# An attention and feed-forward kernel: the high part of two score tiles as two 64-row matmuls, and relu squared in place

## The reference, cut to what matters

```
scores = (1/3136) * z @ z.T            # z: 3136 x 64
attn   = maximum(scores, 0) ** 2
x      = u * (attn @ v)                # v, u: 3136 x 256
h      = maximum(x @ w_in, 0)          # w_in: 256 x 1024
conv   = sum over 3 taps of conv_w[k] * h shifted by k - 1
y      = (h * sigmoid(conv)) @ w_out   # w_out: 1024 x 256
```

## Time and profile before

| what | value |
|---|---|
| median of 2 runs | 1743.33 us (1741.52 to 1745.14) |
| the profiled execution | 1742.73 us |
| its span, first to last instruction | 1740.9 us |
| mean granted TensorE clock | 0.996 |
| matmuls, each with a weight load of its own | 8232 |
| TensorE busy | 1701.0 us |
| DVE, ACT, POOL busy | 1372.0, 1218.1, 196.8 us |

### The profile page before, as it was taken

How to read it: one execution, slowest core, us unless ns; L and a number is a source line. 1 busy time by engine, 2 the same in 40 slices (tenths; PEclk the granted TensorE clock), 3 DMA queues, 4 the chain that set the end, 5 groups by cost and what they waited for, 6 DMA issues and landing times.

```text
span 1740.9 us, 22661 instructions
## 1 busy us (share of the span) xinstructions
PE 1701.0 (98%) x8232; PEld 1548.7 (89%) x8232; DVE 1372.0 (79%) x1826; ACT 1218.1 (70%) x2022; POOL 196.8 (11%) x145
## 2 busy tenths in 40 slices
PE   8899999999999999999999999999999999999996
PEld 7799999988999999998899999999889999999995
DVE  7687778789877878788887788778888777878784
ACT  7667767777776676677777666767776776776664
POOL 7200000024000000003300000000420000000000
PEclk9999999999999999999999999999999999999998
DMA  5100000032000000003200000000310000000000
GB/s 147 53 27 1 27 27 1 27 93 74 1 27 27 1 27 27 27 1 106 62 1 28 27 27 1 27 27 6 112 50 27 1 27 27 1 27 27 22 1 21
DMA packets 28093, 55.34 MB, mean 32 GB/s; under 512 B 2896, under 2 KB 13648, under 8 KB 27984
## 3 DMA queue, kind: packets, MB, share of 16 engines
q1 hardware_dynamic: 27984, 53.90, 10.0%
HBM read 41.04 MB, written 12.85 MB: 31 GB/s over the span
## 4 chain that ended last, share of the span: by engine, by line
PE 88%; DVE 5%; ACT 2%; issue 1%; DMA 0%; POOL 0%; ACTq 0%; DVEq 0%; POOLq 0%
PE ps_h L325 15%; PE ps_av L302 14%; PE ps_av L301 14%; PE ps_av L300 14%; PE ps_y L338 14%; PE ps_s L282 7%; PE ps_s L283 7%; DVE g_sb L583 1%; DVE g_lo L603 1%; DVE attn_lo L544 1%; DVE g_sb L591 1%; PE ps_av L304 1%; PE ps_av L305 1%; ACT attn_hi L410 1%; DMA w_raw<-w_all 0%
## 5 line engine op out<-in xcount | busy, mean ns | idle before, releaser
L556 DVE SCALAR_TENSOR_TENSOR attn<-ps_s,relu_s 128x448 f32<-128x448 f32 x672 | 411.8, 617 | 237.2 <-ACT relu_s L415 236.8
L300 PE MATMUL ps_av<-attn_lo,v_hi 128*128 128x448 f32 x1344 | 494.6, 368 | 10.2 <-DVE attn_lo L544 7.9
L302 PE MATMUL ps_av<-attn_hi,v_lo 128*128 128x448 f32 x1344 | 494.9, 368 | 0.0
L301 PE MATMUL ps_av<-attn_hi,v_hi 128*128 128x448 f32 x1344 | 494.4, 368 | 0.0
L415 ACT ACTIVATE relu_s<-ps_s 128x448 f32<-128x448 f32 x672 | 358.3, 539 | 147.9 <-PE ps_s L283 147.7
L544 DVE TENSOR_TENSOR attn_lo<-attn,attn_hi 128x896 fp32r<-128x896 f32 x336 | 374.7, 1115 | 45.9 <-ACT attn_hi L410 45.4
L410 ACT ACTIVATE attn_hi<-attn 128x896 fp32r<-128x896 f32 x336 | 319.8, 952 | 97.8 <-DVE attn L556 95.9
L300 PEld LDWEIGHTS ps_av<-attn_lo,v_hi 128*128 128x128 f32 x1344 | 252.6, 188 | 37.2 <-issue 15.2
L302 PEld LDWEIGHTS ps_av<-attn_hi,v_lo 128*128 128x128 f32 x1344 | 252.6, 188 | 22.9
L301 PEld LDWEIGHTS ps_av<-attn_hi,v_hi 128*128 128x128 f32 x1344 | 253.0, 188 | 21.9
L282 PE MATMUL ps_s<-z_mv,z_st 128*128 128x448 f32 x672 | 247.1, 368 | 8.2 <-DVE z_st L649 6.5
(11 more groups left out here) (56 smaller groups left out, 1883.3 us busy)
## 6 DMA issues: line engine op xcount, KB each, us to landing
u_sb<-u_win SPq DMA_DIRECT2D x28, 448.0 KB, 4.3
raw<-v_all SPq DMA_DIRECT2D x48, 256.0 KB, 2.7
out<-y_sb SPq DMA_DIRECT2D x24, 448.0 KB, 4.0
z_raw<-z_win SPq DMA_DIRECT2D x28, 224.0 KB, 4.2
raw<-z_all SPq DMA_DIRECT2D x24, 256.0 KB, 2.7
w_raw<-w_all SPq DMA_DIRECT2D x8, 256.0 KB, 2.7
out<-y_sb SPq DMA_DIRECT2D x4, 450.0 KB, 3.2
raw<-v_all SPq DMA_DIRECT2D x4, 128.0 KB, 2.5
```

What stands on the lines that cost most here:

```text
L300: mm(acc, vh, lo, start=j == 0, stop=False)
L301: mm(acc, vh, hi, start=False, stop=False)
L302: done = mm(acc, vl, hi, start=False, stop=False)
L556: dve.scalar_tensor_tensor(dst, scores_bank(j), 0.0, relu_slot(j), ALU.max, ALU.mult).then_inc(attn_ready, 1)
```

## The change

The high x high product of tiles j and j + 1 (j even, up to 23) is now done by two matmuls over 64 rows each: tile j in partitions 0 to 63, tile j + 1 in partitions 64 to 127. The cross products stay matmuls over 128 rows. The order for a pair is: cross product of j, cross product of j + 1, high x high of j, high x high of j + 1, all issued at the step of the even tile; at the odd tile `scores` issues nothing. The low x low product is left out for these tiles. Tile 24 is as before. For the odd tiles the high part must lie in partitions 64 to 127, so ACT rounds them once more into a new tile `z_odd` before it rounds the piece as before (one activation of 64 partitions x 256 elements for each of the 6 full z pieces of a batch), and TensorE waits on a new semaphore `odd_rounded`. `relu_s` is gone: ACT writes relu into the slot of `attn`, and DVE multiplies in place; the wait on `attn_split` moves from DVE to ACT.

```diff
--- before.py
+++ after.py
@@ -125,7 +125,7 @@
         w_lo = sb("w_lo", [P, WPIECES * RAW], F32R)
         taps = sb("taps", [P, TAPS, FT])
 
-        relu_s = sb("relu_s", [P, SBANKS + 1, WIDE])
+        z_odd = sb("z_odd", [P, PAIRS * P], F32R)
         attn = sb("attn", [P, 3, 2, WIDE])
         attn_hi = sb("attn_hi", [P, 3, 2, WIDE], F32R)
         attn_lo = sb("attn_lo", [P, 3, 2, WIDE], F32R)
@@ -157,8 +157,9 @@
 
             return ps_s[:, 0, 0:WIDE] if alone and f % 2 else ps_h[:, 0:WIDE]
 
-        def relu_slot(j):
-            return relu_s[:, j % SBANKS if j < LAST else SBANKS, :]
+        def attn_slot(j):
+
+            return attn[:, j // 2 % 3, j % 2, :] if j < LAST else attn_last[:, :]
 
         z_loaded = sem("z_loaded")
         piece_loaded = [sem(f"piece_loaded{i}") for i in range(RING)]
@@ -195,6 +196,7 @@
         ones_ready = sem("ones_ready")
         zeros_ready = sem("zeros_ready")
         carried = sem("carried")
+        odd_rounded = sem("odd_rounded")
         y_ready = sem("y_ready")
 
         def batch_of(n):
@@ -266,22 +268,36 @@
         def _(pe):
             mm = nc.tensor.matmul
 
-            def scores(n, b, j, first):
-
-                if j == 0:
-                    pe.wait_ge(z_split, n * 2 + 2)
-                if j % ZTILES == 0:
-                    pe.wait_ge(piece_split, b * NP + AT["z", j // ZTILES] + 1)
+            def scores_free(n, j, first):
 
                 if j == LAST:
                     if not first:
                         pe.wait_ge(h_ready, n * FT)
                 elif j >= SBANKS or not first:
                     pe.wait_ge(attn_ready, n * STEPS + j - SBANKS + (1 if j >= SBANKS else 0))
-                w = z_st[:, j * P:(j + 1) * P]
-                mm(scores_bank(j), w, z_mv[:, n % 2, 1, :], start=True, stop=False)
-                mm(scores_bank(j), w, z_mv[:, n % 2, 0, :], start=False, stop=True
-                   ).then_inc(scores_ready, 1)
+
+            def scores(n, b, j, first):
+
+                if j == 0:
+                    pe.wait_ge(z_split, n * 2 + 2)
+                if j % ZTILES == 0:
+                    pe.wait_ge(piece_split, b * NP + AT["z", j // ZTILES] + 1)
+                    if j < LAST:
+                        pe.wait_ge(odd_rounded, b * (LAST // ZTILES) + j // ZTILES + 1)
+                if j == LAST:
+                    scores_free(n, j, first)
+                    w = z_st[:, j * P:(j + 1) * P]
+                    mm(scores_bank(j), w, z_mv[:, n % 2, 1, :], start=True, stop=False)
+                    mm(scores_bank(j), w, z_mv[:, n % 2, 0, :], start=False, stop=True).then_inc(scores_ready, 1)
+                elif j % 2 == 0:
+                    half = P // 2
+                    for k in (j, j + 1):
+                        scores_free(n, k, first)
+                        mm(scores_bank(k), z_st[:, k * P:(k + 1) * P], z_mv[:, n % 2, 1, :], start=True, stop=False)
+                    mm(scores_bank(j), z_st[0:half, j * P:(j + 1) * P], z_mv[0:half, n % 2, 0, :],
+                       start=False, stop=True).then_inc(scores_ready, 1)
+                    mm(scores_bank(j + 1), z_odd[half:P, j // 2 * P:(j // 2 + 1) * P], z_mv[half:P, n % 2, 1, :],
+                       start=False, stop=True).then_inc(scores_ready, 1)
 
             def attend(n, b, j, first):
 
@@ -385,6 +401,10 @@
                 if n is not None and kind == "v":
                     act.wait_ge(attn_used, n * STEPS + v_tiles(k)[-1] + 1)
                 dst = z_st if kind == "z" else v_hi
+                if kind == "z" and cols > P:
+                    odd = z_odd[P // 2:P, k * RAW // 2:k * RAW // 2 + cols // 2].rearrange("p (t c) -> p t c", c=P)
+                    src = raw[P // 2:P, g % RING, 0:cols].rearrange("p (t e c) -> p t e c", e=2, c=P)
+                    act.activation(odd, src[:, :, 1, :], ACT.Copy).then_inc(odd_rounded, 1)
                 act.activation(dst[:, k * RAW:k * RAW + cols], raw[:, g % RING, 0:cols], ACT.Copy
                                ).then_inc(piece_rounded, 1)
 
@@ -412,7 +432,12 @@
             def attention(n, j, first):
 
                 act.wait_ge(scores_ready, n * STEPS + j + 1)
-                act.activation(relu_slot(j), scores_bank(j), ACT.Relu,
+
+                if j == LAST and not first:
+                    act.wait_ge(attn_split, n * ROUNDS)
+                elif j % 2 == 0 and (j >= 6 or not first):
+                    act.wait_ge(attn_split, n * ROUNDS + j // 2 - (2 if j >= 6 else 3))
+                act.activation(attn_slot(j), scores_bank(j), ACT.Relu,
                                scale=1.0 / SEQ / SEQ).then_inc(relu_ready, 1)
                 for back, q in rounds_after(j, ROUND_LAG):
                     if not (first and back):
@@ -547,13 +572,7 @@
             def attention(n, j, first):
 
                 dve.wait_ge(relu_ready, n * STEPS + j + 1)
-
-                if j == LAST and not first:
-                    dve.wait_ge(attn_split, n * ROUNDS)
-                elif j % 2 == 0 and (j >= 6 or not first):
-                    dve.wait_ge(attn_split, n * ROUNDS + j // 2 - (2 if j >= 6 else 3))
-                dst = attn[:, j // 2 % 3, j % 2, :] if j < LAST else attn_last[:, :]
-                dve.scalar_tensor_tensor(dst, scores_bank(j), 0.0, relu_slot(j),
+                dve.scalar_tensor_tensor(attn_slot(j), scores_bank(j), 0.0, attn_slot(j),
                                          ALU.max, ALU.mult).then_inc(attn_ready, 1)
                 for back, q in rounds_after(j, SPLIT_LAG):
                     if not (first and back):
```

More of the change, by code:

```diff
@@ L267, in _ @@
             mm = nc.tensor.matmul
+            def scores_free(n, j, first):
+                if j == LAST:
+                    if not first:
+                        pe.wait_ge(h_ready, n * FT)
+                elif j >= SBANKS or not first:
+                    pe.wait_ge(attn_ready, n * STEPS + j - SBANKS + (1 if j >= SBANKS else 0))
             def scores(n, b, j, first):
```

## The result

The changed kernel takes 1810.89 us (median of 2 runs, 1809.67 to 1812.11) where the one before took 1743.33. The ratio is 1.0383, with a 95% interval of 1.0355 to 1.0412: 3.8% slower. The forecast was 1690 us, and the measured time lies above the range of 1678 to 1790. The rival on the other side, B, names the mechanism; its two prices, 1787 and 1853, lie on both sides of what was measured.

The account below looks back on a forecast made before the run. TensorE was taken to bound ordinary blocks, DVE the ends of batches. 1742.7 - 57 (pairs) + 3 (bank wait) + 1 (rounding) = 1689.7, given as 1690 us with the median 0.6 above the profiled execution; range 1678 to 1790.

Parts of the forecast that it names:

- rival B: Each switch between 128 and 64 rows empties the array: 0.162 us, 1787 in all, 1853 if loads wait; chance 0.25.
- The slot of TensorE: In an ordinary block of 60.18 us TensorE is always busy; each of 294 matmuls takes 0.2047 us.
- Four slots become three: A pair's two 64-row matmuls share one slot, the second 0.015 us later: 0.19 us saved a pair.
- the single unknown: How 64-row matmuls run, absent from the trace; taken as 0.19 us saved a pair.
- The bounds: For a pair's high x high products: from 0.205 us saved at best to 0.354 us lost at worst.
- Rival A: The second 64-row load waits until the first 64-row matmul starts: 0.095 us saved a pair, 1719 us; chance 0.20.
- Rival C: The two 64-row halves don't run side by side, so a pair keeps four slots: 1747 us; chance 0.13.
- How many pairs count: Of 336 pairs, 12 in block 0 and 8 at each of three batch ends left out: 300 pairs, 57 us.
- The odd tile's bank: Wanted a step earlier, it makes TensorE wait at three batch ends: 3 us, bounds 0 and 12.
- the relu in place: ACT's relu waits for the split of three rounds before: no cost; bounds 0 to 1 us at three ends.
- the rounding: 24 extra ACT activations for z_odd, in block 0 and at batch ends: 1 us, bounds 0 and 9.8.
- Chances: 0.45 for faster, 0.23 for slower, 0.32 for within 2%; about 0.15 left out above the range.

Follow-up runs that it names:

- e3: The changed kernel with each cross product followed by its 64-row high x high product, four changes a pair in place of two: 1987.74 us.
- e1: The changed kernel with the high x high products of a pair over 128 rows again, all else kept: 1751.31 us.
- e4: The changed kernel with both 64-row matmuls of a pair in partitions 0 to 63, the same half of the array: 1867.48 us.
- e5: The changed kernel with all three products of a pair's scores as 64-row matmuls, even and odd tile in different halves: 1808.5 us.
- e2: The kernel before with only the multiply in place, relu_s gone and the attn_split wait on ACT: 1744.41 us.
- e9: The kernel of e8 with the stages behind up one step earlier on ACT and DVE: 1718.59 us.
- e7: The kernel of e5 with attend and down in 64-row shared slots too, adding half of each sum twice, for timing only: 1795.85 us.
- e6: The kernel before with down's 12 matmuls as 24 over 64 rows in 12 shared slots, banks swapping halves after a wait: 1826.76 us.
- e10: The kernel of e9 with the last down after everything else in the last step: 1731.95 us.
- e8: The kernel before with all matmuls of blocks 0 to 27 but the last feed-forward over 64 rows, steps in twos, every product complete: 1782.86 us.

## Why the prediction was wrong

*The slot of TensorE.* Right: 294 slots of 0.2047 bound a block, and in every kernel here the slot stayed what it was while the granted clock was 1.00.

*Four slots become three.* The sharing was right: both halves start together, within the same hundredth of a us where I allowed 0.015. The step that failed is the one on the single unknown: "I take 0.19, because the trace shows loads going ahead of matmuls without any gap in every row of the steady stream, and nothing that makes a matmul wait for the end of the one before." All 8232 matmuls of that trace have 128 rows, so it had no row on a change, and the absence was taken for evidence. The runs put in its place 0.19 to 0.20 us lost for each change, 0.38 to 0.40 a pair, against 0.205 saved: +0.18 to +0.19 where the sum had -0.19. The four changes of e3 doubled the price, the undone halves of e1 removed it.

*The bounds and rival B.* The mechanism was there, with its place at both ends of the 64-row pair, and the point from which it decides (0.095 a change). Its price was mis-sized both ways: I had 0.162 without and 0.272 with the load. In fact the next load starts 0.29 us after the start in effect of the last matmul of the other kind, 0.08 after the end of its slot, and then takes its 0.105 uncovered: 0.19. So the load does not wait for the recorded end of the matmul before (0.37 after its start). The changes around the pairs shown of e3, e4 and e5 have 0.28 to 0.30 us at this place, but no run tells why it is 0.08 past the slot. The Trainium skill, page "TensorEngine Tiling (Array Packing)", section "Tiling Modes", says that changing the mode drains TensorE; the trace agrees in that every change costs, 0.19 to 0.20 us, and does not show how far the array is empty by then. I had quoted this rule and still gave its rival a chance of 0.25; it stated the mechanism outright, and the trace had nothing against it.

*Rival A and the loads.* Wrong: the two loads of a shared slot run beside each other (701.76 both). The some 4 ns between starts that the Trainium skill gives in "TensorE: Matmul & The Clock Gate", section "Part 3: Packing small matmuls - row/col tiling", are borne out: in the trace of the changed kernel they are 3 or 4 ns apart in 324 of the 336 pairs. *Rival C* fell with the same rows and with e4: one half for both costs 56.6 us more.

*How many pairs count.* I took off 8 pairs of 24 at each end of a batch as hidden by DVE, and 12 in block 0. That was about right at the ends, for a loss as for a gain. The two blocks at an end, in the changed kernel and in e1, which differ by the halves alone:

```profile
363.54:493.80 130.26, 126.83 (x589) 103.75 (x588) 102.98 (x132) 96.72 (x165) 33.80 (x24) 1.00 0.19 56
349.81:477.19 127.38, 122.36 (x590) 109.80 (x589) 103.19 (x132) 96.08 (x165) 33.96 (x24) 1.00 0.20 57
```

At this first end they differ by 2.88 us where 24 pairs at 0.194 make 4.66, so some 9 pairs are hidden. The sum nearly closes: 65 us for all pairs, less 3 x 1.8 hidden, are the 59.6 us that e1 gives to the halves; with its 7.8 they make 67.4 of the 67.6 us.

*The odd tile's bank, the relu in place, the rounding.* The relu costs nothing, as said (e2). Of the bank wait and the rounding I had 3 + 1 us, within bounds of 0 and 22; e1 measured 7.8 us for the two. The waits of TensorE on DVE's multiply (8.9 us in e1, 0.2 us before) point to the bank for most of it, some 2 us at each end of a batch where I took 1, but no run separates them.

*Chances.* 0.45 for faster and a range ending at 1790 gave the least weight to the one side on which a page named a mechanism and the trace had no row. With bounds of -0.205 and +0.354 a pair, from -69 to +119 us, the range should have reached to its upper end.

## What to carry to other kernels

Matmuls over 64 rows in both halves of the array share one slot, but each change between 64 and 128 rows cost 0.19 to 0.20 us here; so a single saved slot of 0.205 does not pay for going there and back, and two would do so barely (an estimate, 0.41 against 0.38 to 0.40; no run has it). It paid to stay (e9, 24 us less than before): a product over 128 rows can be given as two halves into two banks, crosswise, if each bank changes halves with two slots of other work between. When a trace holds no row for the operation that decides, bound it and keep the range to the bounds; that nothing is seen to wait is no evidence about a case that does not occur.

## What the runs showed that was not expected

- TensorE takes two loads and two matmuls in each 0.205 us over long stretches (e7) and, but for its waits, a whole block (e9), as if they were one of each.
- The busy share of TensorE stayed at 98% while it lost 3.8%: the time lost at a change lies under the recorded length of the matmul before. The 0.29 to 0.30 us "issue" of the loads is the row that shows it.
- Banks handed from one half to the other at once cost 0.42 us in e6, more than the 0.27 worked out from the way out and the load, and 0.34 in e10. Why these two differ is open.
- A pause alone does not tell whether the clock falls. In e8 the wait on g_lo leaves 2.35 us between starts in 23 blocks; behind 18 of them the clock fell to 1.2 GHz, for 1.5 us of loss, and behind 5 it did not. In the changed kernel each end of a batch has a pause of 2.1 us between starts; behind the first two the clock stayed at 1.00, behind the third it fell, and that block is 1.5 us longer than the other two like it (67.5 and 66.0). In the kernel before, the longest there is 1.2 us, and its windows stayed at 1.00. The first and the third end in the changed kernel:

```profile
409.00:413.00 4.00, 2.27 (x11) 1.38 (x10) 4.00 (x7) 3.29 (x5) 0.00 (x0) 1.00 0.23 66
1298.50:1301.50 3.00, 3.00 (x10) 2.66 (x9) 1.68 (x3) 3.00 (x7) 2.28 (x2) 0.50 0.06 9
```
